# A gated recurrence on 64-row matmul tiles, with its second batch's exponentials taken from pre-shifted, pre-masked rows in HBM

## What is computed

```python
# stage 1, per batch and head, token by token
m_new  = max(f[t] + m, i[t])
f_stab = exp(f[t] + m - m_new);  i_stab = exp(i[t] - m_new);  m = m_new
C = f_stab * C + i_stab * outer(v[t], k[t])
n = f_stab * n + i_stab * k[t]
y[t] = sigmoid(o_gate[t]) * (C @ q[t]) / max(abs(n @ q[t]), 1)
# stage 2, x = y with the heads side by side (320 channels)
u = x + (relu(x.T @ w_tok1) @ w_tok2).T
x = u + relu(u @ w_ch1) @ w_ch2
# stage 3
gate = sigmoid(causal depthwise convolution of x, 5 taps)
out  = (gate * (x @ w_val)) @ w_out
```

## Time and profile before

| | us |
|---|---|
| median of 3 runs (lowest to highest) | 289.72 (288.74 to 290.57) |
| the profiled execution, its own time | 291.4 |
| its span, first to last instruction | 289.3 |
| around the span in that execution | 2.1 |

### The profile page before, as it was taken

The page is one execution under the profiler, slowest core; times in us unless marked ns, Lnnn a source line. Parts: engine busy times, 40 slices in busy tenths (PEclk is TensorE's granted clock), DMA queues, the critical chain, the costliest instruction groups (busy, mean ns, idle before and its releaser), DMA issues.

```text
span 289.3 us, 5204 instructions
## 1 busy us (share of the span) xinstructions
PE 264.7 (91%) x1964; PEld 247.3 (85%) x1964; DVE 180.0 (62%) x401; ACT 115.4 (40%) x212; POOL 85.7 (30%) x102
## 2 busy tenths in 40 slices
PE   0598788999999999999999999999999999999675
PEld 0587677679799999999999997899999999999564
DVE  7988877486878568535866303537653168742991
ACT  2664545488444432443432223322232332232731
POOL 4415578903654553155004000000040000130710
PEclk9999999999999999999999999999999999999988
DMA  7699987664765143220000010000000100000101
GB/s 219 155 274 321 302 265 219 212 198 124 208 189 132 57 142 91 84 68 3 0 0 2 3 66 2 0 0 2 0 2 23 45 1 2 0 2 0 56 13 68
DMA packets 26289, 25.68 MB, mean 89 GB/s; under 512 B 13977, under 2 KB 22009, under 8 KB 26265
## 3 DMA queue, kind: packets, MB, share of 16 engines
q1 hardware_dynamic: 21976, 18.72, 22.2%
q10 hardware_dynamic: 4288, 6.64, 7.1%
HBM read 23.34 MB, written 2.02 MB: 88 GB/s over the span
## 4 chain that ended last, share of the span: by engine, by line
PE 74%; DVE 7%; issue 7%; POOL 5%; ACT 4%; DMA 1%; SPq 0%; ACTq 0%; POOLq 0%; DVEq 0%
PE shared L1172 30%; PE h_ps L1306 22%; PE s_ps L1210 4%; PE hv_ps L1191 2%; PE s_ps L1244 2%; PE hv_ps L1195 2%; DVE gate L1039 2%; PE shared L1271 2%; PE h_ps L1244 2%; POOL qs L597 2%; PE shared L1221 1%; DMA mask_sb<-mask 1%; PE shared L1318 1%; DVE prob L930 1%; PE shared L1256 1%
## 5 line engine op out<-in xcount | busy, mean ns | idle before, releaser
L1104 DVE SCALAR_TENSOR_TENSOR h_lo<-shared,h_hi 128x384 fp32r<-128x384 f32 x48 | 26.5, 557 | 40.2 <-ACT h_hi L824 40.1
L1306 PE MATMUL h_ps<-ch_hi,h_hi 128*128 128x320 f32 x144 | 45.4, 315 | 0.0
L1306 PE MATMUL h_ps<-ch_hi,h_lo 128*128 128x320 f32 x144 | 44.5, 309 | 0.0
L824 ACT ACTIVATE h_hi<-shared 128x384 fp32r<-128x384 f32 x48 | 23.1, 488 | 53.2 <-PE shared L1172 50.1
L1306 PE MATMUL h_ps<-ch_lo,h_hi 128*128 128x320 f32 x144 | 44.3, 308 | 0.0
L1172 PE MATMUL shared<-u_hi,ch_hi 128*128 128x384 f32 x96 | 33.1, 344 | 0.1
L1172 PE MATMUL shared<-u_lo,ch_hi 128*128 128x384 f32 x96 | 32.6, 339 | 0.0
L1172 PE MATMUL shared<-u_hi,ch_lo 128*128 128x384 f32 x96 | 32.5, 339 | 0.0
L1210 PE MATMUL s_ps<-q_in,k_in 128*128 128x128 f32 x192 | 27.1, 300 | 3.9 <-DMA q_in<-qT 3.9
L1210 PEld LDWEIGHTS s_ps<-q_in,k_in 128*128 128x128 f32 x192 | 25.2, 211 | 6.1 <-DMA q_in<-qT 4.5
L1039 DVE SCALAR_TENSOR_TENSOR gate<-x,conv_sb,gate 128x384 f32<-128x384 f32 x44 | 29.0, 668 | 1.0
(11 more groups left out here) (181 smaller groups left out, 550.3 us busy)
## 6 DMA issues: line engine op xcount, KB each, us to landing
G_all<-G_scratch SPq DMA_DIRECT2D x11, 512.0 KB, 5.8
o_sig<-on ACTq DMA_DIRECT2D x2, 960.0 KB, 6.7
k_in<-kT SPq DMA_DIRECT2D x24, 80.0 KB
q_in<-qT SPq DMA_DIRECT2D x24, 80.0 KB
kn_in<-kn SPq DMA_DIRECT2D x12, 160.0 KB, 4.3
v_in<-vn SPq DMA_DIRECT2D x12, 160.0 KB, 4.8
stage<-ch ACTq DMA_DIRECT2D x3, 640.0 KB, 4.3
out<-o_sb SPq DMA_DIRECT2D x12, 160.0 KB, 1.8
```

Of the source, the lines that this page charges most:

```text
L824: act.activation(h_hi[i % 3][:], ps_of(key)[:, 0:T], ACT.Relu).then_inc(hi_ready, 1)
L1104: took(dve.scalar_tensor_tensor(out=h_lo[i % 3][:], in0=ps_of(key)[:, 0:T], scalar=0.0, in1=h_hi[i % 3][:].bitcast(F32), op0=ALU.max, op1= ...
L1306: last = pe.matmul(h2_ps[t][:, 0:DM], a[:, tile_cols(t)], w[:, f, :], start=(f == 0 and n == 0), stop=(f == FT - 1 and n == 2))
```

## The change

1. Scores and state products use the 40 rows of a head alone (`r = slice(64 * g, 64 * g + D)`) with groups 0 and 1 taking turns, and `k_in` is half as wide. `apart` is gone; `state` has two buffers and is written once. The `delta` matmuls take turns between the groups too.
2. On PE the state products of a unit come first, then the next unit's scores, then `prob` times values. Token matmuls follow three units behind instead of four.
3. In batch 0, units 2 to 5, DVE makes the exponents of group 0 ahead of the state's addition and those of group 1 behind it, both ahead of `yt`.
4. In batch 1 DVE makes no exponents. HBM holds G of batch 1 in double-width rows, the second half filled with the mask's value (`G_wide`). `skew` copies, HBM to HBM, 128x8 pieces of 512 B for each unit to rows of 4,612 B pitch (`Z_scratch`), so that row p has the masked G of key p; `masked_chunk` loads this into `G_all`. ACT then takes exp with the column of `A_col` as bias, eight instructions of 128x128 for each unit. `decay` of batch 1 is taken once on ACT (`E_row`), stored in HBM, and loaded by broadcast (`decay_chunk`).
5. `exps(NC)`, the exponentials of unit 6, move on ACT from the token mixing to a place ahead of `a_hi`.

```diff
-        k_in = [sb("k_in0", [P, 2, HG * L]), sb("k_in1", [P, 2, HG * L], at=a_at + 4 * S)]
+        k_in = [sb(f"k_in{k}", [P, HG * L]) for k in range(2)]
...
+        decay_in = [sb(f"decay_in{k}", [P, HG * L]) for k in range(2)]
+        E_row = sb("E_row", [B * H, S], at=decay_at)
...
-        state = sb("state", [ROWS, HG * D1])
-        apart = [sb(f"apart{k}", [P, 2, HG * D1]) for k in range(2)]
+        state = [sb(f"state{k}", [ROWS, HG * D1]) for k in range(2)]
...
+        G_wide = nc.dram_tensor("G_wide", [NC, H, 2 * L], F32, kind="Internal").ap()
+        E_dram = nc.dram_tensor("E_scratch", [NC, H * L], F32, kind="Internal").ap()
+        Z_ROW = (H + 1) * L
+        Z_dram = nc.dram_tensor("Z_scratch", [NC, P, Z_ROW], F32, kind="Internal").ap()
...
+            def fill_wide():
+                dst = G_wide[:, :, L:2 * L - 1].rearrange("c h l -> (c h) l")
+                sp.dma_start(dst, mask[P - 1:P, 0:L - 1].broadcast_to([NC * H, L - 1])).then_inc(wide_filled, 16)
+            def fill_masked():
+                for c in range(NC):
+                    sp.dma_start(Z_dram[c, :, 0:L], mask).then_inc(Z_filled, 16)
+            def skew(u):
+                c = u - NC
+                src = bass.AP(tensor=G_wide.tensor, offset=c * H * 2 * L, ap=[[1, P], [2 * L, H], [1, L]])
+                dst = bass.AP(tensor=Z_dram.tensor, offset=c * P * Z_ROW, ap=[[Z_ROW + 1, P], [L, H], [1, L]])
+                sp.dma_start(dst, src).then_inc(Z_made[u % 2], 16)
+            def masked_chunk(u):
+                k, c = u % 2, u - NC
+                if c >= 2:
+                    sp.wait_ge(exp_ready, 2 * (u - 1))
+                else:
+                    sp.wait_ge(expo_ready, 2 * (u - 1))
+                    sp.wait_ge(decay_ready, u - 2)
+                sp.wait_ge(Z_made[k], 16 * (c // 2 + 1))
+                sp.dma_start(G_all[k][:], Z_dram[c, :, 0:H * L]).then_inc(G_in[k], 16)
+            def decay_chunk(u):
...
+                                 E_dram[c:c + 1, g * HG * L:(g + 1) * HG * L].broadcast_to([64, HG * L])
+                                 ).then_inc(decay_loaded[k], 16)
...
-                    sp.dma_start(k_in[k_buffer(u)][64 * g:64 * g + D, g, :],
-                                 kT[u, g]).then_inc(k_loaded[k_buffer(u)], 16)
+                    sp.dma_start(k_in[u % 2][64 * g:64 * g + D, :], kT[u, g]).then_inc(k_loaded[u % 2], 16)
...
-                G_chunk(u)
+                if u < NC:
+                    G_chunk(u)
                 k_chunk(u)
                 q_chunk(u)
-                kn_chunk(u)
+                if u % NC < NC - 1:
+                    kn_chunk(u)
                 v_chunk(u)
+                if u >= NC:
+                    masked_chunk(u)
+                    if u > NC:
+                        decay_chunk(u)
+                    if u + 2 < NU:
+                        skew(u + 2)
...
+                if u == 4:
+                    fill_masked()
                 if u == 5:
                     sp.dma_start(conv_sb[:], conv).then_inc(conv_in, 16)
+                    sp.wait_ge(wide_filled, 16)
+                    sp.wait_ge(Z_filled, 16 * NC)
+                    skew(NC)
+                    skew(NC + 1)
+                    sp.wait_ge(E_made, 1)
+                    sp.dma_start(E_dram.rearrange("c (h l) -> h c l", l=L),
+                                 E_row[H:2 * H, :].rearrange("h (c l) -> h c l", l=L)).then_inc(E_saved, 16)
+                    sp.wait_ge(E_saved, 16)
...
+                decayed = decay_in[k] if b else decay
...
+                if u >= NC:
+                    act.wait_ge(G_in[u % 2], 16 * (u // 2 + 1))
+                    act.wait_ge(hv_ready, u - 1)
+                    for g in range(2):
+                        for j in range(HG):
+                            h = g * HG + j
+                            col = (u - NC) * B * H + H + h
+                            last = act.activation(prob[(2 * u + g) % 4][:, tile_cols(j)], G_all[u % 2][:, tile_cols(h)],
+                                                  ACT.Exp, bias=A_col[:, col:col + 1])
+                        last.then_inc(exp_ready, 1)
+                    return
...
+                    act.wait_ge(G_ready, 2)
+                    act.activation(E_row[:], G_row[:], ACT.Exp).then_inc(E_made, 1)
+                if b == 0 and n + 1 < NC:
                     decays(u + 1)
...
                 attention(0, n)
+            exps(NC)
...
-                        if q == 0 and d == 1:
-                            exps(NC)
...
-                        decays(NC + 1)
...
+                    dve.wait_ge(s_ready, 2 * u + 2)
...
-                        dve.wait_ge(s_ready, w + 1)
                         dve.tensor_tensor(prob[w % 4][:], s_ps[g][:], prob[w % 4][:], ALU.mult).then_inc(prob_ready, 1)
+                spread = b == 0 and 1 <= n < NC - 1
+                if spread:
+                    exponents(u + 1, (0,))
                 if n < NC - 1:
                     key = ("delta", u)
...
-                    new = apart[(u + 1) % 2]
-                    grown(new[0:64, 0, :], slice(0, 64))
-                    last = grown(new[64:ROWS, 1, :], slice(64, ROWS)).then_inc(apart_ready, 1)
-                    if n < NC - 2:
-                        last = grown(state[:], slice(0, ROWS))
-                        took(last, key)
-                    else:
-                        dve.wait_ge(apart_ready, with_next(u))
-                        dve.sem_inc(shared_done[J[key] % 2], 1)
+                    took(grown(state[(u + 1) % 2][:], slice(0, ROWS)), key)
+                if spread:
+                    exponents(u + 1, (1,))
...
+                if b == 0 and n + 1 < NC and not spread:
                     exponents(u + 1)
...
-            exponents(NC, (0,))
...
-                            if k == 0 and d == 0:
-                                exponents(NC, (1,))
-                            elif k == 0:
+                            if k == 0 and d > 0:
...
                 k = u % 2
+                v = u - 1
+                if n >= 1 and v >= 1:
+                    pe.wait_ge(ht_ready, v)
+                if n >= 2:
+                    pe.wait_ge(qs_ready, with_state(v))
+                    done(pe, ("delta", v - 1))
+                    for j in range(HG):
+                        for g in range(2):
+                            r = slice(64 * g, 64 * g + D)
+                            pe.matmul(hv_ps[64 * g:64 * g + D1, tile_cols(j)], state[v % 2][r, j * D1:(j + 1) * D1],
+                                      qs[v % 2][r, tile_cols(j)], start=(j == 0), stop=False)
+                if n < NC:
+                    pe.wait_ge(q_loaded[k], 32 * (u // 2 + 1))
+                    pe.wait_ge(k_loaded[k], 32 * (u // 2 + 1))
+                    if u >= 1:
+                        pe.wait_ge(prob_ready, 2 * u)
+                    for j in range(HG):
+                        for g in range(2):
+                            r = slice(64 * g, 64 * g + D)
+                            last = pe.matmul(s_ps[g][:, tile_cols(j)], k_in[k][r, tile_cols(j)],
+                                             q_in[k][r, tile_cols(j)], start=True, stop=True)
+                            if j == HG - 1:
+                                last.then_inc(s_ready, 1)
                 if n >= 1:
-                    v = u - 1
                     pe.wait_ge(prob_ready, 2 * v + 2)
                     pe.wait_ge(v_loaded[v % 3], 16 * (v // 3 + 1))
-                    if v >= 1:
-                        pe.wait_ge(ht_ready, v)
-                    if n >= 2:
-                        pe.wait_ge(qs_ready, with_state(v))
-                        pe.wait_ge(apart_ready, with_next(v - 1))
                     for j in range(HG):
-                        if n >= 2:
-                            for g in range(2):
-                                pe.matmul(hv_ps[64 * g:64 * g + D1, tile_cols(j)],
-                                          apart[v % 2][:, g, j * D1:(j + 1) * D1], qs[v % 2][:, tile_cols(j)],
-                                          start=True, stop=False)
                         for g in range(2):
                             last = pe.matmul(hv_ps[64 * g:64 * g + D1, tile_cols(j)], v_in[v % 3][:, g * HG + j, :],
-                                             prob[(2 * v + g) % 4][:, tile_cols(j)], start=(n < 2), stop=True)
+                                             prob[(2 * v + g) % 4][:, tile_cols(j)],
+                                             start=(n < 2 and j == 0), stop=(j == HG - 1))
                     last.then_inc(hv_ready, 1)
-                if b == 0 and n >= 4:
-
-                    token_hidden(0, n - 4)
-                if n < NC:
-
```

92 lines of the change are left out of this document (47 added, 45 removed).

## The result

The changed kernel takes 305.88 us (median of 4 runs, 305.05 to 306.59), the kernel before 289.47 beside it: ratio 1.058, 95% interval 1.053 to 1.062. It is 16 us slower. Every ratio here, with its interval, leaves out runs over 1.5% above the lowest of their kernel; medians have all runs. The page of the changed kernel: span, the busy rows of the five engines, and the chain that ended last.

The account below looks back on a forecast made before the run. Loads bound batch 0, TensorE about 67 to 262 us. New wait 5.0 plus clock 1.5, less token mixing 0.8 and batch 1's 7.0, gave -1.3 us: 290.1 profiled, 288.4 as median; range 281.5 to 294.5.

Parts of the forecast that it names:

- The new wait: Ahead of token mixing: ScalarE's exponentials of unit 6 wait for masked G, `a_hi` at 61.6 instead of 56.65, 5.0 us lost.
- Rival (b): Skews before token mixing: HBM-to-HBM pieces at half rate, with the fills 4.7 us more, 293.1 us; chance 0.19.
- Scores pair: Batch 1 on TensorE: two 64-row score matmuls run at once, 1.04 us gained per unit, 6.2 us for six.
- rival (c): Scores on TensorE: weight loads of two row tiles take turns, 6.2 us of gain missing, 294.6 us; chance 0.12.
- State block: State products on TensorE in batch 1: stay paired at 0.94 us; near 0.9, not 1.9, excludes rival (d).
- rival (d): State products in one PSUM bank can't pair from different row tiles, 0.94 us more per unit, 293.1 us; chance 0.06.
- Delta: Batch 1's delta matmuls, 0.70 us, taking turns between groups: 0.25 us gained for each of five units, 1.2 us in all.
- Token mixing: From 58 to 67 us: exponents, exponentials and one `decay` leave VectorE and ScalarE, 0.8 us gained.
- clock: Token mixing: TensorE, idle for 5 us, may run at half clock after it, about 1.5 us lost.
- VectorE in batch 1 at nothing: From 67 us on, taking exponents off VectorE gains nothing by itself, since TensorE doesn't wait for it.
- Batch 0 at nothing: Batch 0: loads set the pace, so score gains are hidden; exponents ahead of `yt` cost up to 1.3 us per unit, covered.
- this sign: Batch 0's end: before 50 us or later than 58 would mean the account of what its loads hide is wrong.

Follow-up runs that it names:

- e5: Changed kernel with all fills and skews issued but read by nobody, batch 1's G loaded by plain broadcast without its mask: 306.2 us, ratio 1.058.
- e12: Changed kernel with the store of E (exp(G) of batch 1) ahead of the skews and batch 1's first exponentials behind the second `u_hi`: 300.8 us, ratio 1.043.
- e3: Changed kernel without fills and skews, batch 1's G loaded by broadcast and its mask left out: 290.6 us, ratio 1.006.
- e4: Changed kernel with skews written at even places (pitch 4608 B instead of 4612), the shift left out: 295.1 us, ratio 1.022.
- e13: Changed kernel with skews written and masked G read at a pitch 64 bytes wider, places at multiples of 64 bytes, shift left out: 297.4 us, ratio 1.029.
- e10: e7 with batch 0's exponents not split but together behind `yt`, against the kernel before: 288.1 us, ratio 0.998.
- e18: Repeat of e10 (exponents not split) on the same chip as e17, against the kernel before: 288.1 us, ratio 0.998.
- e1: Kernel before with row tiles, new TensorE order and split exponents; batch 1's exponents on VectorE and G by broadcast as before: 294.4 us, ratio 1.017.
- e7: e1 with GpSimd in batch 1 waiting for a unit's exponents before its `wv`, against the kernel before: 291.1 us, ratio 0.999.
- e17: Repeat of e7 (split exponents, GpSimd waits) on the same chip as e18, against the kernel before: 290.7 us, ratio 1.005.
- e14: e4 with the copies' reads also from one even place for all rows, shift left out: 297.2 us, ratio 1.026.

## Why the prediction was wrong

288.4 us was said, 305.9 measured, outside the range and with 0.28 on this side.

- **The new wait** (5.0 us) is the step that failed. Its chain was right in kind: store of E behind the skews, SyncE standing, masked G, eight exponentials, `a_hi`. Its sizes were not. The skews, 3.4 us for two at 304 GB/s, cost some 4 each by the estimate above; the fills, 1.3 us, held SyncE's issues for 6.50; the store, put at 52.0, landed at 56.5; a landing of 5.2 became 6.9. `a_hi` came at 68.94 instead of 61.6, beyond my upper bound (9.7 us lost; 12.3 measured).
- **No term for the other loads.** I costed the skews on one chain, and only the first two. e5 shows that the wait for the copies isn't needed, and e12, with both other waits moved, still takes 300.8 us: full engines delay the other loads up to 104 us, weights included. Batch 1, said to take 7.0 us less, took 3.9 more; in e3, without copies, it takes 4.1 less.
- **Rival (b)**, skews at half rate, had the cause, but it was priced for the first two skews and the fills only, at 293.1. It also gave HBM-to-HBM copies as the suspect; e4 and e13 show that such copies at multiples of 64 bytes, with their fills and the masked loads, cost 4.5 to 6.8 us over e3, and the odd places 7.3 to 10.8 more. The fills weren't run apart.
- **Scores pair**: right, 1.09 us for 1.98 (0.89 gained, 1.04 said); rival (c) is out. **State block**: 1.00, not 1.9; rival (d) is out. By the rule that I had named with it (the Trainium skill, TensorEngine Tiling (Array Packing), Gotcha 1: PSUM Pressure) the pairs couldn't run together. Here they do: four pairs take 0.06 us more than the 0.94 said. **Delta**: 0.70 to 0.61, a third of the 0.25 said. **Not in the sum**: the wait for `ht`, 0.35 us a unit, since only delta now stands between the values and the turn. So 0.60 a unit and not 1.2.
- **Token mixing** (-0.8) and **clock** (+1.5): the sum is right. From `a_hi` to the first hidden tile it takes 11.04 us instead of 10.35, the 0.7 more that was said for the two. The split is less sure: TensorE's idle time there falls only from 0.85 to 0.57 us, so the relief looks nearer to 0.3 and the clock nearer to 1. The granted clock in 62 to 67 is 0.56 and in 67 to 72 0.50, behind an idle TensorE, as said. It is also 0.57 in 24 to 32, where I had none. There it costs nothing that is seen: the same kernel has 0.61 in that stretch in e10's profiled execution (288.37 us) and 1.00 in e18's (289.15 us).
- **VectorE in batch 1 at nothing**: too little, it seems. e3 takes 3.7 us less than e1 although its first hidden tile is 3.4 us later: its batch 1 takes 55.48 us, e1's 62.75, e7's 59.23 and e17's 57.65. e3 has no exponents on VectorE there that can meet GpSimd, so the 3.3 us of e7 are probably part of it (argued, not shown).
- **Batch 0 at nothing**: half right. The last token matmul starts at 56.6, between my bounds of 50 and 58, so this sign found nothing. But the split, put down as covered, costs 2.6 us by e17 and e18.

The pieces in ratios to before: row tiles without the split, GpSimd waiting, -0.2%; the split +0.1 and +0.8 in its two pairs; the meeting +1.8 and +1.2; from e1 to e3 (no exponents on VectorE, but the new wait) -1.1; fills, even copies and masked loads +1.6; odd places +3.6. They are the steps of one row of kernels from the one before to the changed one, so they add up to the measured 5.8 whatever they are; the sum is no check on them.

## What to carry to other kernels

Before a copy is added in a stretch where the DMA engines are near full, price it as engine time that every later load pays, and look at where its pieces start: a shift of one element turned 512-byte writes into the largest cost of the change. An order that gains on the bound engine can close a gap that another pair of engines lived on; look for VectorE instructions with two SBUF inputs beside GpSimd's. Undo parts one at a time: what was worth having here was 1.1%, and it was hidden under nearly 6.

## What was not expected of the hardware

Writes of 512-byte pieces, HBM to HBM, take 10.9 us a 512 KB copy at multiples of 4 bytes and 6.7 at multiples of 64; the copies' reads at odd places don't matter (297.4 us with them in e13, 297.2 without in e14). Issuing six 64 KB fills, HBM to HBM, at a DMA share of 0.84 (32 to 40 us), took SyncE 6.50 us. One VectorE instruction of 0.34 us took 3.25 beside GpSimd. Four pairs of 40-row matmuls, on rows 0 and 64 and into one bank, took 1.00 us, nearly as little as pairs from shared rows (0.94).
